# First weights of a fused recurrence and MLP kernel rounded by GpSimd's DMA instead of ScalarE

## The reference

```python
sig = 1.0 / (1.0 + np.exp(-f_logit))
f = lower_bound + (1.0 - lower_bound) * sig
for t in range(S):
    h = f[:, t] * h + (1.0 - f[:, t]) * x[:, t]
    y[:, t] = h
out = np.maximum(y @ w_in, 0.0) ** 2 @ w_out
```

## Time and profile before

| | |
|---|---|
| median of 3 runs | 988.89 us (988.62 to 988.94) |
| profiled execution | 988.73 us |
| its span, first to last instruction | 986.7 us |
| TensorE busy | 982.5 us, 4388 matmuls |
| VectorE, ScalarE, GpSimd busy | 731.9, 697.6, 50.4 us |
| HBM read, written | 29.11 MB, 12.45 MB |

### The profile page before, as it was taken

One profiled execution on the slowest core, in us unless ns is written; L12 is line 12 of the kernel. 1 busy time (PEld: TensorE's weight loads), 2 busy tenths in 40 slices (PEclk: granted clock), 3 DMA queues, 4 the chain that ended last, 5 costly groups with the idle time before them and its releaser, 6 DMA issues.

```text
span 986.7 us, 12612 instructions
## 1 busy us (share of the span) xinstructions
PE 982.5 (100%) x4388; PEld 818.6 (83%) x4388; DVE 731.9 (74%) x940; ACT 697.6 (71%) x925; POOL 50.4 (5%) x50
## 2 busy tenths in 40 slices
PE   9999999999999999999999999999999999999998
PEld 7998888888888888888888888888888888888887
DVE  6997886876777687688688778768768767876545
ACT  8977766766776776776677677677667767766665
POOL 2682000000000000000000000000000000000000
PEclk9999999999999999999999999999999999999999
DMA  9003011002101201100210210110111021001001
GB/s 330 2 13 111 0 44 64 22 1 86 43 1 47 81 0 43 64 21 15 70 43 0 75 52 0 43 64 21 43 43 43 0 85 43 1 0 43 1 1 43
DMA packets 22158, 41.96 MB, mean 43 GB/s; under 512 B 1520, under 2 KB 3056, under 8 KB 22128
## 3 DMA queue, kind: packets, MB, share of 16 engines
q1 hardware_dynamic: 21984, 41.43, 12.1%
q10 hardware_dynamic: 144, 0.13, 0.0%
HBM read 29.11 MB, written 12.45 MB: 42 GB/s over the span
## 4 chain that ended last, share of the span: by engine, by line
PE 100%; DVE 0%; POOL 0%; issue 0%; DVEq 0%; POOLq 0%
PE out_ps L923 52%; PE hidden_ps L908 42%; PE hidden_ps L949 3%; PE out_ps L943 1%; PE out_ps L949 1%; PE out_ps L933 0%; POOL zeros L884 0%; DVE result L844 0%; DVE result L849 0%; DVE result L846 0%; DVEq L848 0%; DVEq L843 0%; POOLq L1200 0%
## 5 line engine op out<-in xcount | busy, mean ns | idle before, releaser
L923 PE MATMUL out_ps<-g_lo,w_out_hi 128*128 128x512 f32 (+1 forms) x760 | 294.1, 387 | 0.0
L923 PE MATMUL out_ps<-g_hi,w_out_lo 128*128 128x512 f32 (+1 forms) x760 | 294.1, 387 | 0.0
L923 PE MATMUL out_ps<-g_hi,w_out_hi 128*128 128x512 f32 (+1 forms) x760 | 294.1, 387 | 0.0
L696 DVE TENSOR_TENSOR g_lo<-h,g_hi 128x1024 fp32r<-128x1024 f32 (+1 forms) x189 | 232.0, 1228 | 64.1 <-ACT g_hi L412 61.1
L405 ACT ACTIVATE h<-h 128x1024 f32<-128x1024 f32 (+1 forms) x189 | 199.3, 1054 | 3.2
L923 PEld LDWEIGHTS out_ps<-g_hi,w_out_hi 128*128 128x128 f32 x760 | 142.7, 188 | 28.3
L923 PEld LDWEIGHTS out_ps<-g_lo,w_out_hi 128*128 128x128 f32 x760 | 142.7, 188 | 28.2
L923 PEld LDWEIGHTS out_ps<-g_hi,w_out_lo 128*128 128x128 f32 x760 | 142.6, 188 | 28.1
L908 PE MATMUL hidden_ps<-sums_hi,wc_hi 128*128 128x512 f32 x352 | 137.0, 389 | 0.0
L908 PE MATMUL hidden_ps<-sums_lo,wc_hi 128*128 128x512 f32 x352 | 137.0, 389 | 0.0
L908 PE MATMUL hidden_ps<-sums_hi,wc_lo 128*128 128x512 f32 x352 | 136.9, 389 | 0.0
(11 more groups left out here) (114 smaller groups left out, 1055.2 us busy)
## 6 DMA issues: line engine op xcount, KB each, us to landing
f_in<-f_logit_t SPq DMA_DIRECT2D x22, 512.0 KB, 4.6
x_in<-x_t SPq DMA_DIRECT2D x22, 512.0 KB, 4.5
out_t<-result SPq DMA_DIRECT2D x20, 512.0 KB, 3.1
w_out_raw<-weights SPq DMA_DIRECT2D x8, 256.0 KB, 6.3
w_in_raw<-weights SPq DMA_DIRECT2D x5, 256.0 KB, 5.9
out_t<-result SPq DMA_DIRECT2D x2, 448.0 KB, 3.0
w_in_raw<-first SPq DMA_DIRECT2D x3, 256.0 KB, 4.0
out_t<-result SPq DMA_DIRECT2D x3, 256.0 KB, 2.0
```

The costliest lines, as they stand in the source:

```text
L696: nc.vector.tensor_tensor(g_lo[b][:, :, 0:n], h_of(it, j, b), g_hi[b][:, :, 0:n].bitcast(F32), ALU.subtract).then_inc(g_ready[b], 1)
L923: mm = nc.tensor.matmul(out_ps[:, b, c, 0:n], half[:, j, m, c * P:(c + 1) * P], moving[b][:, m, 0:n], start=(j == 0 and m == 0 and k == 0) ...
```

## The change

Groups 0 to 2's rounded weights no longer come from ScalarE. GpSimd issues three DMAs that read the same columns of the DRAM array `first` and write `wc_hi`, whose type is fp32r, so that the transfer rounds; it waits for the first load of f before it issues them. The raw weights are still loaded, since the rests and the sums need them, but later in SyncE's order. ScalarE rounds part 0 of y in place of VectorE. Waits on `w_plain_hi_done` become waits on `w_hi_loaded[q]` for groups 0 to 2, and count from group 3 on for the others. The warm-up is 12 matmuls instead of 14.

```diff
-WARM_UP = 14
+WARM_UP = 12
...
+        w_hi_loaded = [sem(f"w_hi_loaded{q}") for q in range(EARLY_QUADS)]
...
             load_part_f(0)
             load_part_x(0)
+            load_part_f(1)
+            load_part_x(1)
+            load_first_f(0)
+            load_first_x(0)
             load_early_w_in(0)
             load_early_w_in(1)
-            load_part_f(1)
+            load_first_f(1)
+            load_first_x(1)
             load_early_w_in(2)
-            load_part_x(1)
-            for c in range(C):
-                load_first_f(c)
-                load_first_x(c)
             load_w_out(0)
...
             for c in range(C):
                 part_forget(0, c)
-            plain_w_in_hi(0)
-            plain_w_in_hi(1)
             part_gate(1)
-            part_forget(1, 0)
-            plain_w_in_hi(2)
-            part_forget(1, 1)
+            for c in range(C):
+                part_y_hi(0, c)
+                part_forget(1, c)
+            gate(0, 1, 0)
             for c in range(C):
                 part_y_hi(1, c)
-            gate(0, 1, 0)
             first_forget(1, 0)
...
             def first_w_in_lo(q):
-                dve.wait_ge(w_plain_hi_done, q + 1)
+                dve.wait_ge(w_hi_loaded[q], 16)
+                dve.wait_ge(w_in_loaded[q], 16)
...
             for c in range(C):
                 part_scan(0, c)
-                part_y_hi(0, c)
...
-                pool.wait_ge(w_plain_hi_done, q + 1)
+                pool.wait_ge(w_plain_hi_done, q - EARLY_QUADS + 1)
...
+            def load_w_in_hi(q):
+
+                begin = first.shape[1] - (EARLY_QUADS - q) * N
+                pool.dma_start(wc_hi[:, q, A11:A21 + 1].rearrange("p b n -> p (b n)"), first[:, begin:begin + N]
+                               ).then_inc(w_hi_loaded[q], 16)
+
             nc.gpsimd.memset(zeros[:], 0.0).then_inc(zeros_done, 1)
+
+            pool.wait_ge(first_f[0][0], 16)
+            for q in range(EARLY_QUADS):
+                load_w_in_hi(q)
             plain_w_in_lo(3)
...
                 def raw_part(k, c, j):
-                    pe.wait_ge(w_plain_hi_done, j + 1)
+                    pe.wait_ge(w_hi_loaded[j], 16)
                     pe.wait_ge(first_hi_done[0][k], c + 1)
...
-                pe.wait_ge(w_plain_hi_done, j + 1)
+                pe.wait_ge(w_plain_hi_done, j - EARLY_QUADS + 1)
...
-        "first": rows(fp[0], bounds, xp[0], w_in[0], w_in[1], fp[1], w_in[2], xp[1]),
+        "first": rows(fp[0], bounds, xp[0], fp[1], xp[1], w_in[0], w_in[1], w_in[2]),
```

More of the change, by code:

```diff
@@ L606, in part_scan @@
                                              ).then_inc(scan_done, 1)
[L608 to L611, removed]
             def part_y_lo(k, c):
```

## The result

The changed kernel takes 994.54 us (median of 6 runs) against 988.84 for the kernel before, a ratio of 1.006 with a 95% interval of 1.0049 to 1.0071: 5.7 us slower, where 989.9 was forecast. Its profiled execution takes 994.52 us with a span of 992.5.

What follows compares the result with a forecast made beforehand. TensorE was taken to bound the kernel, busy 982.5 of 986.7 us, so only its start could move. The profiled 988.73 plus 1.2 for late transfers gave 989.9 us; forecast's own range 989.0 to 990.8, 8-in-10 range 988.5 to 992.8.

Steps and rivals of the forecast that it cites:

- line of 2.0 us: Whole kernel: a difference within 0.2% (2.0 us) was to be called no change.
- rival B: TensorE's early matmuls stay at the lower pace after gaps: 992.8, or 991.3 if the pace doubles halfway; chance 0.22.
- Step 1: TensorE's warm-up ends 0.86 us earlier, at 6.44, worth something only if weights and y are there.
- Step 2: ScalarE's y roundings take 0.55 us each, chunk 1 ready at 7.7; gain 0.0, or 0.1 to 0.2 if short.
- Step 3: GpSimd's three transfers land at 7.6, 8.6 and 9.6, so TensorE's part 1 starts at 11.25, not 10.08: +1.2 us.
- My high end: GpSimd's transfers at the upper bounds: first landing at 10.65, second at 12.0, +4.6 us.
- Step 4: DMA engines carry 0.79 MB more, later loads up to 2.0 us later; no cost under the lag, 0.1 us otherwise.
- Steps 5 and 6: VectorE starts part 1's input at 8.15, not 8.01, covered; SyncE's new load order and GpSimd's issues delay nothing.
- Rival C: VectorE's two-input work holds GpSimd's descriptors until 6.9, first landing at 10.9: +4.4, 993.2; chance 0.08.
- Rival A: GpSimd's transfers are on time, landing by 7.2 and 7.9: 988.7, at best 988.5; chance 0.25.

Runs made afterwards that it cites:

- e6_before_w12: The kernel before with 12 warm-up matmuls in place of 14: 988.8 us, ratio 1.0.
- e4_sp_held: The changed kernel with SyncE's loads from batch 1 on held until the third rounded group has landed: 993.62 us, ratio 1.0058.
- e10_short_hold: The changed kernel with SyncE's loads from batch 1 on held only until x of part 0 has landed, about 4.2 us: 992.71 us, ratio 1.0042.
- e2_no_wait: The changed kernel with GpSimd issuing its transfers at once, at about 1.3 us, without waiting for the first f: 990.08 us, ratio 1.0017.
- e7_before_w6: The kernel before with 6 warm-up matmuls, leaving TensorE idle before the first real matmuls, no transfer differing: 990.79 us, ratio 1.0018.
- e3_dve_held: The changed kernel with VectorE's work on x held until the first rounded weights have landed: 995.87 us in one run.
- e12_early_y_dve: The changed kernel with GpSimd's transfers issued at once, part 0 of y rounded by VectorE and 14 warm-up matmuls: 990.5 us, ratio 1.0014.
- e9_early_held: As e2_no_wait, with SyncE's loads from batch 1 on held until the first group landed and part 1's y rounded before batch 1's tanh: 991.18 us.
- e5_y_on_act: The kernel before with part 0 of y rounded by ScalarE instead of VectorE, the weight casts staying: 989.11 us, ratio 1.0003.

## Why the prediction was wrong, point by point

By the prediction's own line of 2.0 us the result is slower, to which it gave 0.28. That share was also counted a little low: the milder form of rival B, 991.3, lies beyond that line too.

**What bounds the kernel**: right. The loss is one shift of the start, 5.75 us at part 1, and nothing came back later.

**Step 1**, two warm-up matmuls: worth nothing, as e6_before_w12 shows for the kernel before.

**Step 2**, ScalarE: the mechanism was right and the size a little high, 0.50 us for a rounding against my 0.55, and chunk 1 ready at 7.2 in place of 7.7. It was never the bound.

**Step 3 failed.** I gave the first transfer 4.0 us from issue to landing, the median of SyncE's loads of the same size. It took 5.9, the second 7.0, the third 7.8, and the spacing was 1.7 and 1.4 against my 1.0, outside my bounds for it. The issue itself came at 3.90, not 3.65. So the first weights were taken at 9.84 and not at 7.6. The wrong idea was that a queue of GpSimd's own would get its share at once, so that a load early in SyncE's queue was its nearest row. What e4_sp_held, e10_short_hold and e2_no_wait show in its place is that GpSimd's first packet moves up to 1.6 us after the issue with SyncE's queue held, and 3.6 us after it in the changed kernel: the later, the more SyncE has put in ahead. Two rows of before were nearer: batch 1's loads of x, issued at 4.5 and 5.4, 4.6 us, and SyncE's late loads, 6.3 us at the median and 7.0 at most. The 5.9 lies between them. My high end stood at the 7.0, at +4.6 us, and the range left it out.

The estimate that I worked out from the Trainium skill's page DMA: Bandwidth & Descriptors (Anatomy of one DMA), a landing at 7.3, counts the writing of the descriptors twice, since the page's fixed 2.0 us is for setup and completion together. Without that the estimate is 2.6 us from the issue. e4_sp_held, with SyncE's queue held, took 3.2 us and the changed kernel 5.9. So the traces do not agree with the fit, by 0.6 us beside a held queue and by 3.3 beside a full one.

**Step 4**: for e2_no_wait, where TensorE is nearly on time, I would have had 0.1 us for batch 1's late data, and it was 0.2. In the changed kernel they are covered, as I wrote, though VectorE's wait for the raw weights of group 2 was 0.9 us, to 13.25, and not 0.7.

**Steps 5 and 6** cost nothing on the path, as written.

**Rival B** was right in kind, with one difference: in the profiled run the pace had already risen and was then taken back in the gap. It lost 1.5 us and not 2.9. The Trainium skill (TensorE: Matmul & The Clock Gate, Part 1) says that activity releases the clock and idleness takes it back; the trace of the changed kernel (0.50 after the gap) agrees. In e7_before_w6 a broken warm-up put the higher pace off to about 12, as rival B had it. **Rival C** was refuted by e3_dve_held. **Rival A** did not come about, and even with the transfers issued first the time is 990.08 and not 988.7.

**The range** failed for one more reason. I priced the late transfer (+4.6 at its high end) and the lost pace (2.9 on top of 1.2) as separate cases. They are one: the later the weights, the longer the gap, and the gap is what costs the pace. Their sum as measured, 4.2 + 1.5, lies over each of them.

## What to carry to other kernels

In these traces a transfer on a fresh queue did not overtake what the busy queue already held: while the DMA engines are full, price its landing like a load that the busy queue issues at the same moment (here 5.5 to 5.7 us against 5.9), or measure it. When a change can open a gap in TensorE's early work, add the lost pace to the same case, and don't shorten the warm-up on the same bet. A wait in front of such a transfer can cost more than its own length, because the other queue fills meanwhile: here 2.6 us of wait made the first landing 4.2 us later (9.8 against 5.6).

## What was not expected of the hardware

- GpSimd's queue moved no packet for 3.6 us (3.9 to 7.5) beside a busy queue of SyncE, and for 1.6 us at most (3.9 to before 5.5) beside a held one. Once both moved, they shared about evenly: 0.36 MB against SyncE's 0.32 from 8 to 10 us. By which rule the engines choose was not tried.
- The three rounding transfers of 2 KB rows went in 432 packets for 0.79 MB, the plain ones in 240.
- The granted-clock column reads 1.00 at the start although the pace there is the lower one: in e7_before_w6 it does so up to 12 us, with pairs of 256-column matmuls 0.43 apart. In the changed kernel it follows the pace from the first fall on. Before that, the distance between matmuls tells it.
- The moment of the first rise differs from run to run: 12 warm-up matmuls took 4.44 us in the changed kernel's profile and 5.30 in e3_dve_held's, and 14 took 6.05 in the kernel before and 4.52 in e12_early_y_dve.
- Not every gap costs the pace. A wait of 1.0 us (e9_early_held), one of 1.1 (e5_y_on_act), and two of 0.6 and 1.2 close together (e12_early_y_dve) left it at the higher level; waits of 1.7 and 0.6 us close together (e10_short_hold), 1.9 (e4_sp_held) and 4.1 us (the changed kernel) were followed by a fall. These are single profiles, and no rule for the length follows from them.
